# Half steps: a third bank for the first product, packed accumulators, output products three tiles late

## The chip, the cores and the metric

The program runs on one core of a Trainium2 chip. The metric is the device time of one execution in microseconds. The engines are PE (TensorE, matmuls), ACT (ScalarE), DVE (VectorE), POOL (GpSimd) and SP, which here only issues DMAs. Each engine works through its own instruction list in order and waits on semaphores that the others raise.

## The reference, cut to what matters

```
state = 0
for t in range(768):                      # per batch (4) and head (8), head_dim 48
    state = alpha[t][:, None] * state + outer(k[t], v[t])
    y[t] = q[t] @ state
x = y as (3072 tokens, 384)
h = x @ w_in                              # 384 -> 2048
x = (h * cos(h)) @ w_out                  # 2048 -> 384
h = max(x @ w1, x @ w2, x @ w3)           # 384 -> 768
out = h @ w_out2                          # 768 -> 384
```

Everything is float32. Products that need the accuracy are made of three: each operand is split into a high and a low part, and high times high, low times high and high times low are added in PSUM.

## The kernel before

**Tiling.** The sequence is cut into 6 chunks of 128 positions; with 4 batches a chunk has 512 tokens. The attention works in 16 units (4 pairs of heads, 4 batches) for each chunk. The first block of products (h, cos, times `w_out`) goes over 16 tiles of 128 hidden columns for each chunk, and its weights stay in SBUF. The second block follows after the last chunk.

**Half steps.** The attention of chunk c+1 runs beside the products of chunk c. Chunk 0 is special: its products are made in two half steps of 256 tokens each. The first half step (tiles t = 0 to 15) takes the first 256 tokens while the attention units 8 to 15 of chunk 0 and the loading and splitting of the weights still go on; the second (t = 16 to 31) takes the other 256 tokens beside the attention of chunk 1 (`step(0, 0, True, True, True)`). All later steps have 512 tokens for each tile (t = 32 on).

**One tile in a half step.** PE makes `hidden1(t)`: nine matmuls of 256 columns into the bank `h_ps[t % 2]`. ACT then makes `turns` (L558, `turn`), two roundings (L566 and L569, `rounded`), and, after POOL's `frac` (L423), the cosine (L577). DVE multiplies cosine and h into `gated` (L927, `gate`), ACT rounds that to `g_hi` (L584), POOL takes the rest as `g_lo` (L431), and PE makes `accumulate1(t)`: nine matmuls that add to the three output rows `acc[0]`, `acc[1]` (both in `acc_pair`) and `acc[2]` (`acc_last`). `hidden1(t)` waits for `g_done` t-1, that is until gate t-2 has read the bank. PE's list has `accumulate1` two tiles late: hidden(t), accumulate(t-2), then the attention's matmuls of this tile. ACT's list has turn(t), rounded(t), `g_high(t-1)`, cosines(t), and in the first half step a piece of weights (L509) and a copy of states (L517).

**The border between the half steps.** The last accumulates of the first half step (t = 14 and 15) and `stage1(1, 0)` (attention scores of chunk 1) come before hidden(16). Hidden(16) also needs all of x's low part: `x_high0(3)` on ACT (one piece of 96 rows, L529, and three of 32 rows, L537, "quads", two of which ACT makes only after the roundings of tile 15) and `x_low0(3)` on DVE (L860, L874). At the start of the first half step `x_high0(1)` and `x_low0(1)` play the same part, and PE waits for the last of them before hidden(0).

**After the half steps.** ACT copies the three accumulators to `x2` (L721), SP stores it (`spill_x2`). New states of the attention (L839 on DVE) gate the next `stage1` on PE (L1187). SP's list of loads for a chunk a is: queries/keys/decays of pairs 0, 1, 2 (`load_qka`, L270) with the values (`load_v`, L274) between, then the store of x2, then pair 3 and its values.

Of the kernel before, what the change touches and what calls it, by code (L numbers as in the profile page):

```python
# [62 lines left out]
def build(nc, qka, val, wa, wb, spill, out):  # L63
# [8 lines left out]
    with ctx:  # L72
# [47 lines left out]
        with ExitStack() as early:  # L120
# [34 lines left out]
            "mid_state", "y_done", "inc_done", "state_done", "xhi_done", "xlo_done",  # L155
# [24 lines left out]

        def slot(t, half):

            if half:
                tmp, at = t % 2 * HTOK, t // 2 % 2 * HTOK
                return h_ps[t % 2][:, 0:HTOK], slice(tmp, tmp + HTOK), (t % 2, slice(at, at + HTOK)), 2, 4
            bank = last_h[t % 4] if t >= TILES1 * STEPS else h_ps[t % 2]
            return bank[:], slice(0, TOK), (t % 2, slice(0, TOK)), 1, 2
# [75 lines left out]
        def _(sp):  # L263
# [51 lines left out]
            load_qka(1, 3)  # L315
            load_v(1, 2)
            load_v(1, 3)
# [22 lines left out]
            for a in range(2, STEPS):  # L340
                load_qka(a, 0)
                load_v(a, 0)
                load_qka(a, 1)
                load_qka(a, 2)
                load_v(a, 1)
                spill_x2(a - 2)
                load_qka(a, 3)
                load_v(a, 2)
                load_v(a, 3)
            low_ready(sp, POOL_W - 1)  # L350
# [134 lines left out]
        def _(act):  # L485
# [34 lines left out]
            def x_high0(g):  # L520
# [7 lines left out]
                else:  # L528
                    nc.scalar.activation(x_hi[0:PAIR_E, 0, 2, half], y_ps[0:PAIR_E, 0:HTOK],  # L529
                                         ACT.Copy).then_inc(S["xhi_done"], 1)  # L530
                    x_high0_quads(g, (0,))

            def x_high0_quads(g, quads):

                half = slice(g // 2 * HTOK, (g // 2 + 1) * HTOK)
                for j in quads:
                    nc.scalar.activation(x_hi[PAIR_E:P, 0, j, half], y_ps[QUAD * j:QUAD * (j + 1), HTOK:TOK],  # L537
                                         ACT.Copy).then_inc(S["xhi_done"], 1)
# [65 lines left out]
            x_high0_quads(1, (1, 2))  # L604
# [3 lines left out]
            for i in range(TILES1):  # L608
# [11 lines left out]
                if last:  # L620
                    x_high0_quads(3, (1, 2))
# [60 lines left out]

            def step(c, s, attend, prepare_next, half):
                for i in range(TILES1):
# [34 lines left out]
                wait(act, "spilled", 16 * c)  # L719
                for j in range(KT):  # L720
# [48 lines left out]
        def _(dve):  # L769
# [84 lines left out]
            def x_low0_quads(g, quads):  # L854

                half = slice(g // 2 * HTOK, (g // 2 + 1) * HTOK)
                before = g // 2 * (XHI - 1) + g % 2
                for j in quads:
                    dve.wait_ge(S["xhi_done"], before + 2 + j)
                    nc.vector.tensor_tensor(x_lo[0][PAIR_E:P, j, half], y_ps[QUAD * j:QUAD * (j + 1), HTOK:TOK],  # L860
                                            x_hi[PAIR_E:P, 0, j, half].bitcast(fp32), ALU.subtract)

            def x_low0(g):
# [8 lines left out]
                else:  # L872
                    x_low0_quads(g, (1, 2))
                    last = nc.vector.tensor_tensor(x_lo[0][0:PAIR_E, 2, half], y_ps[0:PAIR_E, 0:HTOK],  # L874
                                                   x_hi[0:PAIR_E, 0, 2, half].bitcast(fp32), ALU.subtract)
                    last.then_inc(S["xlo_done"], 1)
# [40 lines left out]
            x_low0_quads(1, (0,))  # L917
# [37 lines left out]
            for i in range(TILES1):  # L955
# [4 lines left out]
                if i == TILES1 - 1:  # L960
                    x_low0_quads(3, (0,))
                elif i in ahead0:
# [5 lines left out]
                if i == TILES1 - 1:  # L968
                    x_low0(3)
                    scan(*ahead0[i])  # L970
# [203 lines left out]
        def _(pe):  # L1174
# [44 lines left out]
            def split_mm(ps, w_at, x_pair, first, final):  # L1219

                xh, xl = x_pair
                mm(ps, w_hi[:, w_at], xh, start=first, stop=False)  # L1222
# [242 lines left out]
```

## Time and profile before

| what | value |
|---|---|
| median of 3 runs | 876.67 us (874.59 to 877.75) |
| the profiled execution's own time | 877.27 us |
| its span (first to last instruction) | 875.3 us |
| PE busy | 832.8 us (95%) |
| DVE, ACT, POOL busy | 69%, 50%, 27% |
| mean granted TensorE clock | 0.988 |
| first half step, hidden(0) to hidden(16) | 33.45 to 99.88 us |
| second half step, hidden(16) to hidden(32) | 99.88 to 161.06 us |

A row of the timeline gives the start, the duration, the engine, the line, what is written and read, and in brackets how long the engine had been idle before and what ended that. Neighbouring matmuls overlap, so starts tell more than durations. The second view of the profile's page cuts the span into 40 slices; after the eighth slice PE stands at 9 tenths or more in every one.

### The profile page before, as it was taken

How to read it: one execution, taken by the hardware profiler on the slowest of the kernel's cores; microseconds unless marked ns; L12 is line 12 of the kernel's file. 1: busy time of each engine (PE TensorE's matmuls, PEld its weight loads, DVE VectorE, ACT ScalarE, POOL GpSimd, SP SyncE). 2: the span in 40 equal slices, each digit the busy share in tenths (PEclk: the TensorE clock that was granted, in tenths of full speed). 3: DMA queues.
4: the chain of work that ended last, by engine and by line, in shares of the span. 5: the costliest groups of instructions: out<-in, count | busy, mean ns of one | idle time of the engine just before them, and what ended most of it. 6: DMA issues, size and time to landing. Idle time of an engine off the chain costs nothing.

```text
span 875.3 us, 15696 instructions
## 1 busy us (share of the span) xinstructions
PE 832.8 (95%) x5446; PEld 759.8 (87%) x5446; DVE 601.6 (69%) x1254; ACT 435.1 (50%) x944; POOL 235.7 (27%) x274
## 2 busy tenths in 40 slices
PE   4687799999999999999999999999999999999998
PEld 4677798888888888888888888889999999999998
DVE  8578588777777777777677457757756566556454
ACT  3686576644454445444544446646343434434333
POOL 6575455333324332333233213310000000000000
PEclk9699899999999999999999999999999999999999
DMA  9632132312321131223123001130101000100001
GB/s 254 178 100 75 35 94 72 113 32 55 82 77 42 55 82 64 55 55 82 64 55 134 3 37 37 40 114 28 38 37 37 37 37 27 31 15 36 1 37 37
DMA packets 13781, 54.36 MB, mean 62 GB/s; under 512 B 1968, under 2 KB 2480, under 8 KB 13712
## 3 DMA queue, kind: packets, MB, share of 16 engines
q1 hardware_dynamic: 12992, 49.55, 19.2%
q0 software_dynamic: 720, 3.93, 1.1%
q8 instruction: 38, 0.62, 0.3%
q14 instruction: 31, 0.25, 0.1%
HBM read 44.04 MB, written 9.44 MB: 61 GB/s over the span
## 4 chain that ended last, share of the span: by engine, by line
PE 48%; DVE 1%; ACT 1%; issue 0%; POOL 0%; DVEq 0%; ACTq 0%
PE h_ps L1315 4%; PE score L1315 4%; PE h_ps L1317 4%; PE h_ps L1316 4%; PE score L1317 4%; PE score L1316 4%; PE h_ps L1222 2%; PE h_ps L1224 2%; PE h_ps L1223 2%; PE acc_pair L1222 2%; PE acc_pair L1223 2%; PE acc_pair L1224 2%; PE acc_pair L1296 1%; PE acc_pair L1295 1%; PE acc_pair L1297 1%; PE acc_last L1224 1%
## 5 line engine op out<-in xcount | busy, mean ns | idle before, releaser
L423 POOL TENSOR_TENSOR work<-work 128x512 f32<-128x512 f32 (+1 forms) x107 | 119.9, 1121 | 307.0 <-DVE work L941 259.3
L577 ACT ACTIVATE work<-work 128x512 f32<-128x512 f32 (+1 forms) x112 | 63.6, 568 | 138.1 <-POOL work L423 131.6
L1222 PE MATMUL h_ps<-x_hi,w_hi 128*128 128x512 f32 (+1 forms) x312 | 121.0, 388 | 5.1 <-DVE work L927 2.7
L927 DVE TENSOR_TENSOR work<-work,h_ps 128x512 f32<-128x512 f32 (+1 forms) x104 | 62.8, 604 | 85.2 <-ACT work L577 84.6
L1224 PE MATMUL h_ps<-x_lo,w_hi 128*128 128x512 f32 (+1 forms) x312 | 113.5, 364 | 0.0
L1223 PE MATMUL h_ps<-x_hi,w_lo 128*128 128x512 f32 (+1 forms) x312 | 113.0, 362 | 0.0
L1222 PE MATMUL acc_pair<-g_hi,w_hi 128*128 128x512 f32 (+1 forms) x224 | 84.2, 376 | 14.6 <-POOL g_lo L431 14.3
L808 DVE RECIPROCAL inv_decay<-decay 112x128 f32<-112x128 f32 x96 | 90.2, 943 | 0.5
L584 ACT ACTIVATE g_hi<-work 128x512 fp32r<-128x512 f32 (+1 forms) x112 | 63.5, 567 | 47.9 <-DVE work L927 42.8
L1224 PE MATMUL acc_pair<-g_lo,w_hi 128*128 128x512 f32 (+1 forms) x224 | 81.7, 365 | 0.0
L1223 PE MATMUL acc_pair<-g_hi,w_lo 128*128 128x512 f32 (+1 forms) x224 | 81.7, 365 | 0.0
L558 ACT ACTIVATE work<-h_ps 128x512 f32<-128x512 f32 (+1 forms) x104 | 54.7, 526 | 48.5 <-PE h_ps L1224 47.6
L480 POOL DMA_DIRECT2D out<-raw x5 | 2.9, 575 | 256.8 <-DVE raw L1117 256.8
L933 DVE TENSOR_TENSOR g_lo<-work,g_hi 128x512 fp32r<-128x512 f32 x80 | 61.9, 774 | 13.9 <-ACT g_hi L584 12.4
L1222 PEld LDWEIGHTS h_ps<-x_hi,w_hi 128*128 128x128 f32 x312 | 60.3, 193 | 12.6 <-DVE work L927 3.1
L1224 PEld LDWEIGHTS h_ps<-x_lo,w_hi 128*128 128x128 f32 x312 | 59.9, 192 | 9.7
L1223 PEld LDWEIGHTS h_ps<-x_hi,w_lo 128*128 128x128 f32 x312 | 60.3, 193 | 7.1
L1222 PEld LDWEIGHTS acc_pair<-g_hi,w_hi 128*128 128x128 f32 x224 | 42.6, 190 | 24.9 <-POOL g_lo L431 15.4
L1315 PE MATMUL h_ps<-x_hi,w_hi 128*128 128x256 f32 x216 | 61.5, 285 | 0.0
L1315 PE MATMUL score<-x_hi,w_hi 128*128 128x256 f32 x216 | 61.4, 284 | 0.0
L1317 PE MATMUL score<-x_lo,w_hi 128*128 128x256 f32 x216 | 60.4, 280 | 0.0
L1317 PE MATMUL h_ps<-x_lo,w_hi 128*128 128x256 f32 x216 | 60.4, 280 | 0.0
(205 smaller groups left out, 2409.5 us busy)
## 6 DMA issues: line engine op xcount, KB each, us to landing
v_all<-val SPq DMA_DIRECT2D x24, 576.0 KB, 3.9
raw<-qka SPq DMA_DIRECT2D x46, 288.0 KB, 5.0
block_out<-x SPq DMA_DIRECT2D x6, 768.0 KB, 3.3
x_in<-block_out SPq DMA_DIRECT2D x6, 768.0 KB, 4.4
raw<-wb SPq DMA_DIRECT2D x12, 384.0 KB, 3.1
out<-raw POOLq DMA_DIRECT2D x5, 768.0 KB, 3.6
stage_own<-wa SPq DMA_DIRECT2D x6, 384.0 KB, 6.8
x<-wa SPq DMA_DIRECT2D x6, 384.0 KB, 5.5
```

Source lines behind the costliest of these rows:

```text
L423: nc.gpsimd.tensor_tensor(frac[:, cols], turns[:, cols], whole[:, cols], ALU.subtract).then_inc(S["frac_done"], 1)
L577: nc.scalar.activation(cosine[:, cols], frac[:, cols], ACT.Sin, scale=TURN).then_inc(S["cos_done"], 1)
L584: nc.scalar.activation(g_hi[:, odd, at], gated[:, cols], ACT.Copy).then_inc(S["ghi_done"], 1)
L808: nc.vector.reciprocal(inv_decay[R, s, b], decay[R, s, b]).then_inc(S["inv_done"], 1)
L927: nc.vector.tensor_tensor(gated[:, cols], cosine[:, cols], h, ALU.mult).then_inc(S["g_done"], 1)
L933: nc.vector.tensor_tensor(g_lo[:, odd, at], gated[:, cols], g_hi[:, odd, at].bitcast(fp32), ALU.subtract).then_inc(S["glo_done"], 1)
L1222: mm(ps, w_hi[:, w_at], xh, start=first, stop=False)
L1223: mm(ps, w_lo[:, w_at], xh, start=False, stop=False)
L1224: return mm(ps, w_hi[:, w_at], xl, start=False, stop=final)
L1315: mm(ps, hi, x_h, start=start, stop=False, skip_group_check=grown)
L1316: mm(ps, lo, x_h, start=False, stop=False, skip_group_check=grown)
L1317: return mm(ps, hi, x_l, start=False, stop=stop, skip_group_check=grown)
```

## The change

1. **Banks.** In a half step hidden(t) no longer alternates between two banks. `half_bank` gives three: `h_ps[0]`, `h_ps[1]` and `acc[2]` in the first half step; `acc[0]`, `h_ps[0]`, `h_ps[1]` from t = 19; t = 16 to 18 alternate between the two `h_ps`. The wait becomes `g_done` t-2 (gate t-3), with t = 17 and 18 as before.
2. **Accumulators.** Half an accumulator is 256 columns, so `half_acc` packs two into a bank: first half step `acc[0]` front and back and `acc[1]` front; second `acc[2]` front and back and `acc[1]` back.
3. **Lateness.** `accumulate1` comes three tiles late, and accumulate(14) and (15) come after hidden(16) and hidden(17).
4. **Copies.** `copy_half(0)` reads the first half step's sums into `x2` on ACT after cosines(18); hidden(19) waits for it (`x2_half`), since it writes `acc[0]`. At the end `copy_half(1)` stands in place of the three copies of 512 columns.
5. **x's parts.** Hidden(0) and hidden(16) wait row by row (`x_row`) for x's low part, no longer for all of it. `x_high0(3)` is made in one go before turn(15), and `x_low0(3)` directly after gate(14).
6. **Loads.** SP's order has pair 3 ahead of the store of x2, and `load_qka(a+1, 0)` ahead of `load_v(a, 3)`, `load_qka(a+1, 1)` ahead of `load_v(a+1, 0)`.

```
+        def half_bank(t):
+            if t < TILES1:
+                return (*h_ps, acc[2])[t % 3]
+            if t < TILES1 + 3:
+                return h_ps[(t + 1) % 2]
+            return (acc[0], *h_ps)[(t - TILES1) % 3]
...
+            def copy_half(part):
+                pair, at = (acc[0], acc[2])[part], slice(part * HTOK, (part + 1) * HTOK)
+                nc.scalar.activation(x2[:, 0:2, at], pair.rearrange("p (j n) -> p j n", j=2), ACT.Copy).then_inc(S["x2_half"], 1)
+                return nc.scalar.activation(x2[:, 2, at], acc[1][:, at], ACT.Copy)
...
+                    if half and i == 2:
+                        act.wait_ge(S["acc_done"], TILES1)
+                        low_ready(act, TILES1 - 1)
+                        copy_half(0).then_inc(S["x2_half"], 1)
...
-                if t < TILES1 * STEPS + 2:
-                    wait(pe, "g_done", t - 1)
+                if t == 2:
+                    pe.wait_ge(S["state_done"], 2 * 6)
+                if t == TILES1 + 3:
+                    pe.wait_ge(S["x2_half"], 2)
+                elif half:
+                    wait(pe, "g_done", {TILES1 + 1: TILES1, TILES1 + 2: TILES1 + 1}.get(t, t - 2))
...
+                    if half and i == 0:
+                        if k < KT - 1:
+                            pe.wait_ge(S["x_row"], (KT - 1) * (t // TILES1) + k + 1)
+                        else:
+                            pe.wait_ge(S["xlo_done"], 2 * (t // TILES1) + 2)
...
-                lag = 2 if attend else 3
+                lag = 3 if half or not attend else 2
...
+                    if half and i < 2:
+                        accumulate1(TILES1 - 2 + i, TILES1 - 2 + i, 0, half)
```

PE's list at the border, before. Rows are in PE's order; `acc_pair<-g_hi` begins an accumulate, `h_ps<-x_hi` a hidden product, `score` is the attention's stage1.

```order
L1187 MATMUL score<-q_dec,k_split 128x128 [waits state_done,mask_done,split_done]
...
L1222 MATMUL acc_pair<-g_hi,w_hi 128x256 [waits glo_done]
...
L1222 MATMUL acc_last<-g_hi,w_hi 128x256
...
L1222 MATMUL h_ps<-x_hi,w_hi 128x256 [waits g_done,xlo_done]
...
L1187 MATMUL score<-q_dec,k_split 128x128 [waits state_done,mask_done]
```

These are stage1(1, 0), accumulate(15) with its third row, hidden(16) and stage1(1, 1). PE's list at the same place now, up to the wait for the copy:

```order
L1234 MATMUL h_ps<-x_hi,w_hi 128x256 [waits xlo_done]
...
L1234 MATMUL acc_pair<-g_hi,w_hi 128x256 [waits glo_done]
...
L1213 MATMUL y_ps<-scores,v_all 96x128 [waits mask_done,xlo_done,v_in0]
...
L1234 MATMUL h_ps<-x_hi,w_hi 128x256 [waits g_done]
...
L1228 MATMUL score<-v_all,scores 112x96 [waits mask_done]
L1234 MATMUL acc_pair<-x_hi,w_hi 128x256 [waits x2_half]
```

Hidden(16), of which the third row's wait is shown, now stands ahead of accumulate(14); hidden(17) follows; and hidden(19), which writes `acc_pair`, has a wait of its own for ACT's copy.

ACT's list around the end of the first half step, before, where x's high parts (`x_hi<-y_ps`) stand against the work of tile 15:

```order
L529 ACTIVATE x_hi<-y_ps 96x256 [waits y_done]
L537 ACTIVATE x_hi<-y_ps 32x256
L558 ACTIVATE work<-h_ps 128x256 [waits cos_done,h_done]
L566 ACTIVATE work<-work 128x256 [waits frac_done,turns_done]
L569 ACTIVATE work<-work 128x256 [waits up_done]
```

and now:

```order
L544 ACTIVATE x_hi<-y_ps 96x256 [waits y_done]
L547 ACTIVATE x_hi<-y_ps 32x256 x3
L568 ACTIVATE work<-h_ps 128x256 [waits cos_done,h_done]
L576 ACTIVATE work<-work 128x256 [waits frac_done,turns_done]
L579 ACTIVATE work<-work 128x256 [waits up_done]
```

All three pieces of 32 rows are now ahead of turn(15).

## Rows read from the trace of the kernel before

**Rows 1.** Waits, whole span, PE: us in total, times, longest.

```profile
PE acc_pair L1222 <- POOL g_lo L431: 14.3, 14, 3.2
```

**Rows 2.** Waits, ACT, both half steps (30 to 160 us).

```profile
ACT work L577 <- POOL work L423: 17.0, 25, 1.6
ACT work L558 <- PE h_ps L1224: 12.8, 11, 4.2
```

**Rows 3.** Timeline, ACT, tile 6: turn and cosine.

```profile
57.17 0.38 ACT L558 ACTIVATE work<-h_ps 128x256 f32<-128x256 f32 x1
...
59.30 0.42 ACT L577 ACTIVATE work<-work 128x256 f32<-128x256 f32 x1 [0.54 <-POOL work L423]
```

**Rows 4.** Timeline, start of the first half step: DVE, PE, POOL, ACT.

```profile
31.68 1.29 DVE L860 TENSOR_TENSOR x_lo<-y_ps,x_hi 32x256 fp32r<-32x256 f32 x3 [1.22 <-ACT x_hi L537]
32.98 0.42 DVE L874 TENSOR_TENSOR x_lo<-y_ps,x_hi 96x256 fp32r<-96x256 f32 x1
...
33.45 0.39 PE L1222 MATMUL h_ps<-x_hi,w_hi 128*128 128x256 f32 x1 [2.40 <-DVE x_lo L874]
...
36.67 0.73 POOL L423 TENSOR_TENSOR work<-work 128x256 f32<-128x256 f32 x1 [1.12 <-ACT work L569]
...
37.43 0.42 ACT L577 ACTIVATE work<-work 128x256 f32<-128x256 f32 x1 [0.84 <-POOL work L423]
```

**Rows 5.** Waits, ACT, 60 to 90 us.

```profile
ACT work L558 <- PE h_ps L1224: 1.3, 2, 0.6
```

**Rows 6.** Timeline, ACT at the border: turn(15), g_high(15), turn(16).

```profile
91.53 0.38 ACT L558 ACTIVATE work<-h_ps 128x256 f32<-128x256 f32 x1
...
96.52 0.42 ACT L584 ACTIVATE g_hi<-work 128x256 fp32r<-128x256 f32 x1 [2.16 <-DVE work L927]
...
102.04 0.38 ACT L558 ACTIVATE work<-h_ps 128x256 f32<-128x256 f32 x1 [4.25 <-PE h_ps L1224]
```

**Rows 7.** Timeline, PE at the border: accumulate(14), hidden(16), hidden(19).

```profile
94.35 0.39 PE L1222 MATMUL acc_pair<-g_hi,w_hi 128*128 128x256 f32 x1 [3.17 <-POOL g_lo L431]
...
99.88 0.41 PE L1222 MATMUL h_ps<-x_hi,w_hi 128*128 128x256 f32 x1
...
109.98 0.36 PE L1222 MATMUL h_ps<-x_hi,w_hi 128*128 128x256 f32 x1
```

**Rows 8.** Busy time by window: PE, PEld, DVE, ACT, POOL, granted clock, DMA.

```profile
95.50:102.30 6.80, 5.64 (x28) 5.38 (x27) 3.48 (x9) 1.47 (x5) 0.72 (x1) 0.50 0.01 4
102.40:109.20 6.80, 6.14 (x57) 5.95 (x56) 5.34 (x14) 5.22 (x16) 5.25 (x8) 1.00 0.00 0
44.30:95.40 51.10, 39.79 (x328) 37.45 (x328) 39.05 (x70) 37.98 (x98) 31.60 (x41) 1.00 0.33 90
```

**Rows 9.** Timeline, ACT: turn(18), cosine(18); and the copies to x2.

```profile
107.46 0.36 ACT L558 ACTIVATE work<-h_ps 128x256 f32<-128x256 f32 x1
...
110.25 0.42 ACT L577 ACTIVATE work<-work 128x256 f32<-128x256 f32 x1
...
161.06 1.09 ACT L721 ACTIVATE x<-acc_pair 128x512 f32<-128x512 f32 x2 [0.99 <-PE acc_last L1224]
```

**Rows 10.** Timeline, PE, second half step: hidden(22), accumulate(20), hidden(23).

```profile
120.48 0.36 PE L1222 MATMUL h_ps<-x_hi,w_hi 128*128 128x256 f32 x1
...
121.63 0.28 PE L1222 MATMUL acc_pair<-g_hi,w_hi 128*128 128x256 f32 x1
...
123.92 0.36 PE L1222 MATMUL h_ps<-x_hi,w_hi 128*128 128x256 f32 x1
```

**Rows 11.** Timeline, stalls of the second half step: PE, DVE, PE; then hidden(32).

```profile
133.78 0.46 PE L1187 MATMUL score<-q_dec,k_split 112*128 112x128 f32 x2 [0.65 <-DVE state L839]
...
134.71 0.77 DVE L792 TENSOR_TENSOR_SCAN decay<-raw,ones 112x63 f32<-112x63 f32 x1 [0.63 <-DMA raw<-qka]
...
158.08 0.39 PE L1222 MATMUL acc_pair<-g_hi,w_hi 128*128 128x256 f32 x1 [1.01 <-POOL g_lo L431]
...
161.06 0.50 PE L1222 MATMUL h_ps<-x_hi,w_hi 128*128 128x512 f32 x1
```

More of the change, by code:

```diff
@@ L179, in banks, with half_acc @@
             return score[n % 2], inc_ps[n % 2], 2, 2
+        def half_bank(t):
[4 more added lines that the diff above has]
+            return (acc[0], *h_ps)[(t - TILES1) % 3]
+        def half_acc(t):
+            front, back = slice(0, HTOK), slice(HTOK, TOK)
+            if t < TILES1:
+                return acc[0][:, front], acc[0][:, back], acc[1][:, front]
+            return acc[2][:, front], acc[2][:, back], acc[1][:, back]
         def slot(t, half):
@@ L338, in load_weights2 @@
                 sp.dma_start(stage2[at], wb[n, at]).then_inc(S[f"stage2_in{at}"], 16)
[L340 to L346, printed above, removed]
+            for a in range(1, STEPS):
                 load_qka(a, 3)
+                if a > 1:
+                    spill_x2(a - 2)
                 load_v(a, 2)
+                if a < STEPS - 1:
+                    load_qka(a + 1, 0)
                 load_v(a, 3)
+                if a < STEPS - 1:
+                    load_qka(a + 1, 1)
+                    load_v(a + 1, 0)
+                    load_qka(a + 1, 2)
+                    load_v(a + 1, 1)
             low_ready(sp, POOL_W - 1)
@@ L530, in x_high0 @@
                                          ACT.Copy).then_inc(S["xhi_done"], 1)
[L531 to L538, printed above, removed]
+                    for j in range(KT):
+                        nc.scalar.activation(x_hi[PAIR_E:P, 0, j, half], y_ps[QUAD * j:QUAD * (j + 1), HTOK:TOK],
+                                             ACT.Copy).then_inc(S["xhi_done"], 1)
             act.wait_ge(S["init_dve"], 1)
@@ L719, in step @@
                 wait(act, "spilled", 16 * c)
+                if half:
+                    copy_half(1).then_inc(S["x2_done"], 1)
+                    return
                 for j in range(KT):
@@ L852, in x_low_quad @@
                     last.then_inc(S["xlo_done"], 1)
[L854 to L861, printed above, removed]
             def x_low0(g):
@@ L871, in x_low0 @@
                                             x_hi[to].bitcast(fp32), ALU.subtract).then_inc(S["xlo_done"], 1)
[L872 to L876, printed above, removed]
+                    return
+                for j in range(KT):
+                    dve.wait_ge(S["xhi_done"], before + 2 + j)
+                    last = nc.vector.tensor_tensor(x_lo[0][PAIR_E:P, j, half], y_ps[QUAD * j:QUAD * (j + 1), HTOK:TOK],
+                                                   x_hi[PAIR_E:P, 0, j, half].bitcast(fp32), ALU.subtract)
+                    if j < KT - 1:
+                        last.then_inc(S["x_row"], 1)
+                nc.vector.tensor_tensor(x_lo[0][0:PAIR_E, 2, half], y_ps[0:PAIR_E, 0:HTOK],
+                                        x_hi[0:PAIR_E, 0, 2, half].bitcast(fp32),
+                                        ALU.subtract).then_inc(S["xlo_done"], 1)
             def low_weights(k):
@@ L1241, in hidden1, with accumulate1 @@
                 last.then_inc(S["h_done"], 1)
-            def accumulate1(t, i, tok, copied, half):
+            def accumulate1(t, i, copied, half):
                 _, _, (odd, at), _, _ = slot(t, half)
@@ L1249, in accumulate1 @@
                     w_at = i * W1COLS + KT * P + j * P
-                    last = split_mm(acc[j][:, tok], slice(w_at, w_at + P), (g_hi[:, odd, at], g_lo[:, odd, at]),
-                                    i == 0, i == TILES1 - 1)
+                    to = half_acc(t)[j] if half else acc[j]
+                    shared = half and j == 1
+                    last = split_mm(to, slice(w_at, w_at + P), (g_hi[:, odd, at], g_lo[:, odd, at]),
+                                    i == 0 and not shared, i == TILES1 - 1, half and j < 2)
                 last.then_inc(S["acc_done"], 1)
@@ L1379, in step @@
                         increment(c + 1, i)
-                if not attend:
+                if lag == 3:
                     accumulate(last - 2)
```

43 lines of the change are left out of this document (17 added, 26 removed).

## The prediction

> **What bounds the kernel now.** I read the engines' busy shares first: PE has 95% of the span, and from the end of the half steps on it is all but continuous. So time can only be won or lost in the first 161 us, and what is won there reaches the end only if the later steps start earlier by it, since they are PE's own work, which the change leaves alone.
>
> In the half steps the waits of PE name POOL's low part in front of an accumulate: 14.3 us in 14 waits [rows 1]. That is what "three tiles late" and "a third bank" aim at. But a wait of PE costs time only where the next thing that PE makes is itself late for somebody. So the second view is ACT's waits: over both half steps ACT waits 17.0 us for POOL's fraction, and 12.8 us for a hidden product [rows 2]. The timeline then shows why these are to be kept apart. In a typical tile of the first half step turn(6) starts at 57.17 and the cosine at 59.30, with 0.54 us of waiting for POOL between [rows 3]: ACT starts a turn, makes two roundings and g_high, waits for the fraction, makes the cosine, then weights and states, and goes straight to the next turn, without any wait for PE. From turn(6) at 57.17 to turn(15) at 91.53 it takes 34.36 us for 9 tiles, 3.8 us each [rows 3, 6]. PE needs for a tile twice nine matmuls, and nine take 1.15 us (121.63 less 120.48), so 2.3 us, and about 0.5 us of attention on average, estimated from the 1.14 that the full attention of a tile takes there (3.44 less 2.3) [rows 10]. So **the first half step is bound by ACT's order with its bubble at POOL**, and the 14.3 us of PE are slack for the most part. The **second half step is bound by PE**: hidden(22) to hidden(23) takes 3.44 us with no idle time [rows 10].
>
> **The change part by part.** Times are those of the profiled execution. I follow hidden(0), turn(15), turn(16), hidden(19) and hidden(32).
>
> *Start.* Before, hidden(0) waits for all of x's low part, until 33.45. The three rows of it are written from 31.68 to 32.97 and the rest by 33.40 [rows 4]. Now two thirds of hidden(0) are made while the last parts are written, and only its last three matmuls follow at 33.45. That brings turn(0) forward by about 1.3 us. POOL had been idle for 1.12 us before its first fraction at 36.67, so it can follow by that much at most, and the cosine at 37.43 moves by 1.05 us or so [rows 4]. Bounds 0 and 1.3, taken **-1.05**.
>
> *First half step.* ACT's order is unchanged up to tile 15, so what goes is its waits for PE: 1.3 us, two of 0.6 [rows 5]; **-1.3**. The rest of PE's 14.3 us brings nothing here. Bounds -0.9 (POOL or DVE is next, see the 0.54) and -2.5 (some of DVE's work, masks above all, moves forward with PE and POOL's fraction comes a little sooner).
>
> *Border.* Turn(15) to turn(16) took 10.51 us (91.53 to 102.04), of which ACT waited 2.16 for gate(15) and 4.25 for hidden(16) [rows 6]. PE had made accumulate(14) at 94.35 after 3.17 us idle, and hidden(16) could only begin at 99.88 [rows 7]. Now hidden(16) stands ahead and is through by about 94. The price: two more quads ahead of turn(15), 0.8 us; but they stood in the place of the wait for the fraction before, so I charge 0.5. Then cosine(15), gate(15) (no longer behind x's low part, a scan and an inverse), g_high(15), states and mid_state follow one another, and turn(16) can start at 96.6 on this scale, 4.65 for that chain after turn(15) plus small gaps. 102.04 - 96.6 = **-5.4**. Bounds -4.25 (only the wait for hidden(16) goes) and -6.4 (both waits go).
>
> *The wait for the copy.* This is the one wait that the change adds. The stretch from turn(16) to turn(18) took 5.42 us, and cosine(18) came 2.79 after turn(18) [rows 6, 9], so cosine(18) comes at 96.6 + 5.65 + 2.8 = 105.05 (with 0.2 for hidden(18), which must await gate(16)). copy_half(0) reads 512 and 256 columns: 512 columns cost 0.55 (1.09 for two [rows 9]), so both some 0.92. Hidden(19) then starts at 105.05 + 0.35 + 0.92 = 106.35, and PE has been idle for about 3 us, since its list to there (hidden 17, 18, accumulate 14, 15 and three units) is done by 103.2. Queued behind it on PE are accumulate(16) and the attention of unit 4; ACT waits for hidden(19) a good 1 us at turn(19). Before, hidden(19) began at 109.98 [rows 7], so PE stands 3.63 us better at hidden(19), of which 5.4 are the border's and -1.8 this wait's: **+1.8**.
>
> *The moved accumulate.* PE had made accumulate(16) before hidden(19); now it has not, and the second half step is PE's: **+1.05** (nine matmuls, 1.15 less the first one's fill [rows 10]).
>
> *The rest of the second half step.* From 109.98 to 161.06 PE was stalled 0.65, 0.54 and 0.67 for new states and 1.01 for the low part of tile 30 (the first and the last are in [rows 11], the other two are like the first). The first and the third stand behind DVE's order (x's low part, then a scan and small operations) and stay. The second came after DVE had waited 0.63 us for a load of keys that SP had queued behind `load_v(1, 3)`; the new order of loads sends it some 5 us earlier, so it goes. The last goes, and about 0.25 comes back, since accumulate(31) still needs its chain from hidden(31). Sum -0.54 - 1.01 + 0.25 = **-1.3**. The last copies to x2 are shorter, 0.92 for 1.65; PE doesn't wait for them: 0. The loads of later chunks pass each other while their own conditions are met tiles earlier: 0.
>
> *The clock.* Right after the longest idle time of PE, the 3.17 us up to 94.35, the granted clock was at half from 95.5 to 102.3; in the 51 us before, with most of PE's other, shorter waits in them, it stayed at 1.00 [rows 1, 7, 8]. The new gap of 3 us ahead of hidden(19) is of that size, and behind it PE is the bound, so every matmul at 1.2 GHz in place of 2.4 counts. A fall of 6.8 us costs half of it, 3.4, none costs 0. The old gap was followed by further waits, the new one by steady work, so I take the middle, a fall half as long: **+1.7**.
>
> Sum: -1.05 - 1.3 - 5.4 + 1.8 + 1.05 - 1.3 + 1.7 = **-4.5**. I round the profiled 877.27 to 872.8; against the median of 876.67 that is **872.2** (the profiled one is 0.6 above the median, well inside the spread of the three). The bounds of the terms together reach from about -9 to +0.
>
> **Rivals.**
>
> (a) *No fall of the clock after the copy's gap*, because three matmul groups of the border stand close together before it. Then the +1.7 goes: 870.5. For it: the gaps from 44.3 to 95.4 cost no clock [rows 8]. Against: the gap of 3.17 did.
>
> (b) *The gain is eaten.* The clock stays at half for 6.8 us as before (+1.7 more) or PE's stalls on new states grow, as the accumulates no longer give DVE time: four sites in the second half step (units 1, 5, 9, 13) of 0.65 where there are three; and the start gives nothing. -4.5 + 1.7 + 1.0 = -1.8: 874.9, no change that can be told (0.3%, 2.6 us, is about what a measurement of this kernel can tell from none).
>
> (c) *DVE becomes the bound of the second half step.* Its order for a unit (new state, gate, scan, inverse, mask) has 5.34 busy of 6.80 in the window after the border [rows 8], 2.7 for 3.44, and PE's stall at 133.78 shows it late once [rows 11]. With PE 4 to 5 us further on and without slack, each DVE delay by POOL's traffic would fall on a stage1. It decides once DVE needs more than 3.44 us for a tile on the mean; at 3.9 the 13 tiles from hidden(19) on give 13 x 0.46 = 6.0 more, and -4.5 + 6.0 = +1.5; with a clock that falls in the gaps (1.7 more): +3.2, 879.9. This is the slower end. Against it: the mean of the trace is 2.7.
>
> (d) *The clock oscillates in the first half step.* With three banks PE runs ahead, then stops at each tile for gate t-3. Its idle time there is the same in sum (11.3 of 51.1 us, [rows 8]). A fall of 6.8 us takes 3.4 x 0.78 (the busy share of that window) = 2.65 us of PE's work, of which PE's slack of 1.0 a tile (3.8 less 2.8) covers 1.8: 0.85 for each. Four falls give +3.4: 875.6. The Trainium skill names this (TensorE: Matmul & The Clock Gate, "A second HAM failure mode: psum-queue depth-cycling"): cycling through PSUM banks lets PE idle briefly so often that the clock goes up and down. By that rule this case would come about; the trace of before, with two banks in turn and a dozen gaps, shows a full clock for 51 us and speaks against it.
>
> (e) *It does more*: masks and gates come earlier and shorten POOL's and ACT's bubbles in the first half step, and there is no fall: -8, 868.7.
>
> **Chances.** The forecast 0.38; (a) 0.22; (b) 0.16; (c) 0.06; (d) 0.06; (e) 0.12. Faster by over 0.3%: the forecast, (a) and (e), and about nothing of the others: 0.72. Within 0.3%: (b) and most of (d): 0.21. Slower: (c) and 0.01 for what I don't see: 0.07. The range runs from 867.5, just beyond (e), to 876.5, which holds (b) and (d), and leaves (c) out.
>
> **What would show each step.** Start: the first hidden product in three pieces, cosine(0) near 36.4. First half step: ACT with no wait for a hidden product, PE's waits moved from the low part to `gated`, turn(15) some 2.3 us earlier less 0.8 for the quads. Border: turn(16) about 5 us after turn(15). Copy: PE idle for about 3 us before a hidden product that writes `acc_pair`, started by ACT's copy; hidden(19) at about 104; a half clock behind it. Second half step: 3.44 us a tile, two stalls on new states, none by a load. Hidden(32) near 156.5. The prediction is wrong if the first half step gets shorter by more than 3 us (then ACT's order was not its bound), if turn(16) comes later than 6.5 us after turn(15), or if the gap before hidden(19) is under 1 or over 5 us.

## The result

The changed kernel takes 870.96 us (median of 20 runs, 870.14 to 877.07), the kernel before 876.12 in the same runs. The ratio is 0.9943, 95% interval 0.9928 to 0.9959: about 5 us faster. The profiled execution has a span of 870.7 us against 875.3.

Five moments of the two traces show where. Times are the starts of the instructions named.

| moment | before | after | the stretch up to it: before, after |
|---|---|---|---|
| cosine(0) | 37.43 | 36.02 | |
| turn(15) | 91.53 | 89.75 | 54.10, 53.73 |
| turn(16) | 102.04 | 93.94 | 10.51, 4.19 |
| hidden(19) | 109.98 | 105.26 | 7.94, 11.32 |
| hidden(32) | 161.06 | 156.15 | 51.08, 50.89 |
| end of the span | 875.3 | 870.7 | 714.2, 714.5 |

The waits of PE over the whole span, after (us in total, times, longest), answer to [rows 1]:

```profile
PE score L1199 <- ACT k_split L559: 18.7, 4, 13.0
PE acc_pair L1234 <- POOL g_lo L446: 2.9, 2, 1.7
PE acc_pair L1234 <- ACT x L694: 2.7, 1, 2.7
...
PE score L1199 <- DVE state L859: 1.9, 5, 0.6
PE h_ps L1234 <- DVE work L942: 1.8, 1, 1.8
```

The kernel before has one wait of the first kind, at the start of the kernel:

```profile
PE score L1187 <- ACT k_split L549: 13.0, 1, 13.0
```

The wait for the low part has shrunk from 14.3 us in 14 waits to 2.9 in 2. Those 11.4 us are not the gain. Half of them came back under another name: PE now runs ahead and stands 5.7 us, in three waits, before attention scores, until ACT has split the keys. The waits of ACT in both half steps answer to [rows 2]:

```profile
ACT work L587 <- POOL work L438: 17.8, 26, 2.0
ACT work L568 <- PE h_ps L1236: 7.2, 9, 1.3
ACT work L568 <- PE acc_pair L1236: 2.5, 3, 1.2
...
ACT work L568 <- PE acc_last L1236: 0.6, 1, 0.6
```

A hidden product now lies in one of three tiles, so its wait has three rows: 10.3 us together for 12.8. The longest was 4.2 and is now 1.3: that is the border. The wait for POOL's fraction is about as large as before, 17.8 for 17.0.

The border, ACT, after (answers to [rows 6]): the quads, turn(15), cosine(15), g_high(15), mid_state, turn(16).

```profile
88.56 1.17 ACT L547 ACTIVATE x_hi<-y_ps 32x256 fp32r<-32x256 f32 x3
89.75 0.38 ACT L568 ACTIVATE work<-h_ps 128x256 f32<-128x256 f32 x1
...
91.87 0.42 ACT L587 ACTIVATE work<-work 128x256 f32<-128x256 f32 x1 [0.53 <-POOL work L438]
92.77 0.42 ACT L594 ACTIVATE g_hi<-work 128x256 fp32r<-128x256 f32 x1 [0.49 <-DVE work L942]
...
93.94 0.38 ACT L568 ACTIVATE work<-h_ps 128x256 f32<-128x256 f32 x1
```

Turn(16) follows without any wait. PE at the same place and at the copy (answers to [rows 7]): first row of hidden(16), accumulate(14), and hidden(19), which now goes into `acc_pair`.

```profile
89.53 0.36 PE L1234 MATMUL h_ps<-x_hi,w_hi 128*128 128x256 f32 x1 [0.22 <-DVE x_lo L886]
```

```profile
92.58 0.39 PE L1234 MATMUL acc_pair<-g_hi,w_hi 128*128 128x256 f32 x1 [1.17 <-POOL g_lo L446]
```

```profile
105.26 0.39 PE L1234 MATMUL acc_pair<-x_hi,w_hi 128*128 128x256 f32 x1 [2.75 <-ACT x L694]
```

And busy time and clock around that (columns as in [rows 8]):

```profile
99.90:106.70 6.80, 4.05 (x37) 3.89 (x36) 5.24 (x13) 4.86 (x13) 3.58 (x6) 1.00 0.40 87
106.80:110.20 3.40, 3.40 (x20) 3.40 (x19) 0.47 (x1) 1.77 (x5) 1.41 (x2) 0.50 0.00 0
110.30:117.10 6.80, 6.80 (x65) 6.80 (x64) 5.91 (x18) 4.60 (x12) 3.54 (x6) 1.00 0.26 89
```

PE stands idle for 2.75 us, and a half clock of 3.4 us follows: 20 matmuls in 3.4 us, where the next window of twice that length has 65.

### The profile page after: what moved, and what is told of

The parts are those of the page before. It is cut to its first block, busy times and chain, and to the rows that moved or that the text cites. A ratio compares the mean times of both kernels' runs of the same rounds, so it can differ in the third digit from the quotient of the medians.

```text
span 870.7 us, 15698 instructions
## 1 busy us (share of the span) xinstructions
PE 832.6 (96%) x5446; PEld 760.9 (87%) x5446; DVE 601.1 (69%) x1254; ACT 435.1 (50%) x945; POOL 236.3 (27%) x274
## 4 chain that ended last, share of the span: by engine, by line
PE 48%; DVE 1%; ACT 1%; issue 0%; POOL 0%; DVEq 0%; ACTq 0%
PE h_ps L1338 4%; PE score L1338 4%; PE h_ps L1340 4%; PE h_ps L1339 4%; PE score L1340 4%; PE score L1339 4%; PE h_ps L1234 2%; PE h_ps L1236 2%; PE h_ps L1235 2%; PE acc_pair L1234 2%; PE acc_pair L1235 2%; PE acc_pair L1236 2%; PE acc_pair L1320 1%; PE acc_pair L1319 1%; PE acc_pair L1318 1%; PE acc_last L1235 1%
## 5 line engine op out<-in xcount | busy, mean ns | idle before, releaser
L1234 PE MATMUL h_ps<-x_hi,w_hi 128*128 128x512 f32 (+1 forms) x282 | 111.9, 397 | 3.8 <-DVE work L942 1.8
L942 DVE TENSOR_TENSOR work<-work,h_ps 128x512 f32<-128x512 f32 (+1 forms) x94 | 58.6, 624 | 81.3 <-ACT work L587 80.9
L1236 PE MATMUL h_ps<-x_lo,w_hi 128*128 128x512 f32 (+1 forms) x282 | 104.7, 371 | 0.0
L1235 PE MATMUL h_ps<-x_hi,w_lo 128*128 128x512 f32 (+1 forms) x282 | 104.2, 370 | 0.0
L568 ACT ACTIVATE work<-h_ps 128x512 f32<-128x512 f32 (+1 forms) x94 | 50.9, 541 | 42.3 <-PE h_ps L1236 41.5
L1234 PEld LDWEIGHTS h_ps<-x_hi,w_hi 128*128 128x128 f32 x282 | 54.2, 192 | 11.6 <-DVE work L942 2.0
L1236 PEld LDWEIGHTS h_ps<-x_lo,w_hi 128*128 128x128 f32 x282 | 53.8, 191 | 9.7
L1339 PE MATMUL h_ps<-x_hi,w_lo 128*128 128x256 f32 x216 | 60.4, 280 | 0.0
L1339 PE MATMUL score<-x_hi,w_lo 128*128 128x256 f32 x216 | 60.4, 280 | 0.0
```

Source lines behind the costliest of these rows:

```text
L942: nc.vector.tensor_tensor(gated[:, cols], cosine[:, cols], h, ALU.mult).then_inc(S["g_done"], 1)
L1234: mm(ps, w_hi[:, w_at], xh, start=first, stop=False, skip_group_check=shared)
L1235: mm(ps, w_lo[:, w_at], xh, start=False, stop=False, skip_group_check=shared)
L1236: return mm(ps, w_hi[:, w_at], xl, start=False, stop=final, skip_group_check=shared)
L1339: mm(ps, lo, x_h, start=False, stop=False, skip_group_check=grown)
```

## The experiments

Theory A is the one of the prediction: the first half step is bound by ACT's order, with its bubble at POOL's fraction; the gain is made at the border; the copy's wait and the half clock behind it give part of it back. Rival B: PE's waits for the low part were the loss, and the third bank and the lateness in the first half step are the gain. Rival C: the second half step is held by DVE's and ACT's chains. Rival D: ACT is only just the bound, POOL or DVE is next.

The table has, for each, the time, the ratio to the kernel before (interval in brackets), and moments of the profiled execution. The first four ran on one chip, the next four on another, the last three on a third.

| kernel | median us | ratio | turn(15) | turn(16) | hidden(19) | hidden(32) | span |
|---|---|---|---|---|---|---|---|
| the change again | 871.56 | 0.9930 [0.9904, 0.9956] | 89.80 | 93.99 | 105.29 | 155.24 | 869.8 |
| two banks in the first half step | 872.45 | 0.9952 [0.9931, 0.9974] | 91.47 | 95.66 | 106.92 | 157.70 | 872.3 |
| old border | 874.39 | 0.9964 [0.9940, 0.9988] | 90.34 | 98.67 | 108.08 | 157.70 | 872.2 |
| early copy | 869.08 | 0.9926 [0.9899, 0.9952] | 90.28 | 94.48 | 101.44 | 151.90 | 866.5 |
| old loads | 873.12 | 0.9962 [0.9947, 0.9977] | 90.75 | 94.94 | 104.73 | 156.95 | 871.4 |
| filled bubble | 867.21 | 0.9900 [0.9872, 0.9929] | 87.04 | 91.24 | 101.03 | 151.86 | 866.1 |
| both | 865.93 | 0.9885 [0.9863, 0.9907] | 87.03 | 91.22 | 98.17 | 149.33 | 863.8 |
| all rows waited for | 872.42 | 0.9950 [0.9936, 0.9964] | 90.47 | 94.67 | 106.00 | 156.08 | 870.6 |
| busy gap | 877.42 | 1.0016 [1.0007, 1.0025] | 88.62 | 92.81 | 104.12 | 153.53 | 875.4 |
| both, again | 867.32 | 0.9889 [0.9872, 0.9907] | 85.82 | 90.01 | 96.95 | 148.11 | 862.4 |
| more filled | 866.75 | 0.9887 [0.9873, 0.9902] | 87.06 | 91.25 | 99.41 | 150.91 | 865.5 |

The moments of one kernel differ from run to run by a us or so, since the clock falls at different moments in the attention ahead of the first half step. Differences between moments of one run are steadier: from hidden(32) to the end all kernels but "busy gap" take 714.2 to 714.6 us. What a kernel wins up to hidden(32) thus reaches the end.

**The change again.**

> The changed kernel once more, as the partner of the others on the same chip. Both theories: 0.9943 of the kernel before, some 5 us faster, with PE idle for 2.5 to 3 us before hidden(19).

It repeats to 0.1 us up to hidden(19), 2.75 us of waiting there included.

**Two banks and two tiles in the first half step, the border as changed.**

```
             if t < TILES1:
-                return (*h_ps, acc[2])[t % 3]
+                return h_ps[t % 2]
...
-                if i >= 3:
-                    accumulate1(i - 3, i - 3, 0, True)
+                if i >= 2:
+                    accumulate1(i - 2, i - 2, 0, True)
```

> The changed kernel with two banks and accumulates two tiles late in the first half step, and the rest of the change kept (hidden(16) and (17) ahead of accumulate(14) and (15), packed accumulators, three banks and three tiles from hidden(19) on). Theory A (the first half step is bound by ACT's order, the gain is made at the border): 0 to 1.3 us slower than the changed kernel, about 871.5. Rival B (the third bank and the later accumulates of the first half step bring the gain, as PE's 14.3 us of waits suggest): 3 us slower or more, 874 and up. Either way PE's waits for the low part in front of an accumulate come back.

Turn(15) comes 1.7 us later than in the run of the changed kernel beside it, although cosine(0) came 0.9 earlier (35.21 for 36.08): the stretch between them takes 56.3 us for 53.7, so it is 2.5 longer. The spans are 2.5 apart and the means of the runs 2.1 (873.1, 871.1), but the medians only 0.9, as the twelve runs spread from 870.7 to 877.4. PE, 30 to 90 us:

```profile
PE acc_pair L1234 <- POOL g_lo L446: 6.8, 10, 1.4
```

The waits for the low part are back (6.8 us in 10; the changed kernel has 1.7 there in 1), and the kernel is some 1 to 2.5 us slower. That lies between theory A's 0 to 1.3 and rival B's 3, and this run alone does not decide between them. ACT has the cost in these rows (same stretch):

```profile
ACT work L587 <- POOL work L438: 11.5, 15, 1.6
ACT state L532 <- PE score L1228: 1.8, 1, 1.8
ACT work L568 <- PE h_ps L1236: 1.7, 3, 0.7
```

3.5 us of waiting for PE, where the changed kernel has 1.2 (below): these 2.3 us make up nearly all of the 2.5. Of PE's waits only the part counts that reaches ACT; that is theory A's kind of term, but larger than its 1.3. It is not what the banks brought over the kernel before, which took 54.1 us for the stretch, or 54.9 with the two quads that the change puts into it. Why two banks are slower here than they were there stays open.

**The old border alone.**

```
+            accumulate1(TILES1 - 2, TILES1 - 2, 0, True)
             stage1(1, 0)
+            accumulate1(TILES1 - 1, TILES1 - 1, 0, True)
...
-                    if half and i < 2:
-                        accumulate1(TILES1 - 2 + i, TILES1 - 2 + i, 0, half)
```

> The changed kernel with the old border alone: accumulate(14), stage1(1, 0) and accumulate(15) again ahead of hidden(16); three banks, row-wise waits, loads and copies as changed. Theory A: the border's 5.4 us come back, less the 1.8 of the copy's wait (the first sums are then ready early and the copy is not late) and the moved accumulate (1.05), so 3 to 5 us slower than the changed kernel, 874 to 876. Rival B: under 1 us slower, 871 to 872.

2.8 us slower than the changed kernel on the same chip, and none of its 12 runs (873.35 to 875.87) reaches the slowest of the other's 7 (871.79). ACT's wait at turn(16) is back at once:

```profile
98.67 0.38 ACT L568 ACTIVATE work<-h_ps 128x256 f32<-128x256 f32 x1 [4.18 <-PE h_ps L1236]
```

Turn(15) to turn(16) takes 8.33 us for 4.19. From turn(16) to turn(18) it takes 5.41 for 7.30, since the half clock at the border now falls into ACT's wait, so 2.25 of the 4.14 us are left at hidden(19). (The 1.05 us of the expectation are not undone by this edit: accumulate(16) still comes after hidden(19).) The loss of 2.8 is a little under the 3 to 5 expected, but more than half of the 5 us gained, and rival B, with under 1, falls.

**The copy ahead of turn(18).**

```
+                    if half and i == 2:
+                        act.wait_ge(S["acc_done"], TILES1)
+                        low_ready(act, TILES1 - 1)
+                        copy_half(0).then_inc(S["x2_half"], 1)
                     turn(t, half)
...
                     cosines(t, half)
-                    if half and i == 2:
-                        ...
```

> The changed kernel with ACT's copy of the first sums moved from behind cosine(18) to ahead of turn(18). Theory A's price for the copy's wait is 1.8 us for the idle time of PE before hidden(19) and 1.7 us for the half clock behind it. If it holds, PE no longer stands still there, the clock stays at full and the kernel gets 3 to 4.5 us faster, 866.5 to 868. Rival C (the second half step is held by DVE's and ACT's chains, not by PE, so that PE's gap is slack): no more than 1 us faster, 870 to 871.

2.5 us faster than the changed kernel by the medians, 3.3 by the spans; three of its ten runs lie at 872.7 to 874.9, so the times alone don't settle it, and the trace has to. The copy is made while ACT would have waited for hidden(18), and hidden(19) starts without a wait:

```profile
99.89 0.57 ACT L693 ACTIVATE x<-acc_pair 128x512 f32<-128x512 f32 x1
100.37 0.37 ACT L694 ACTIVATE x<-acc_pair 128x256 f32<-128x256 f32 x1
100.64 0.38 ACT L568 ACTIVATE work<-h_ps 128x256 f32<-128x256 f32 x1
```

```profile
101.44 0.36 PE L1234 MATMUL acc_pair<-x_hi,w_hi 128*128 128x256 f32 x1
```

Hidden(19) is 3.85 us earlier than in the run beside it, and the half clock behind it is gone. From turn(16) to hidden(19) it takes 6.96 us for 11.30. Not all of that is the copy's: this run has no half clock at the border either, and without it the changed order takes 9.79 ("old loads", "filled bubble"). So the copy's place is worth 2.8 us there. But from there to hidden(32) it takes 50.46 us, no less than the 49.95 of the run beside it, though that had a half clock in it. PE's waits of this kernel, 94 to 155 us:

```profile
PE score L1199 <- DVE state L859: 1.5, 2, 1.1
```

1.5 us of waits for DVE's states came back, 1.1 and 0.4 at 108 and 112 us. So the second half step is PE's, as theory A has it, but with so little to spare on DVE that what the missing half clock gives PE is lost there; there is something in rival C.

**The old order of loads.**

```
-            for a in range(1, STEPS):
-                load_qka(a, 3)
-                if a > 1:
-                    spill_x2(a - 2)
...
+            for a in range(2, STEPS):
+                load_qka(a, 0)
+                load_v(a, 0)
```

> The changed kernel with the old order of loads on SP. Theory: the load of keys for chunk 2 is again queued behind a load of values, DVE waits about 0.6 us for it at the scan in tile 25 and 0.2 in tile 29, and one of PE's stalls on a new state of about 0.5 us comes back: 0.5 us slower than the changed kernel, not to be told by the time (871 to 872), but to be seen in the trace. Rival: the old order is harmless because the loads are early enough when the second half step starts sooner: no such wait.

DVE's waits for the keys are back, and larger:

```profile
130.21 0.78 DVE L812 TENSOR_TENSOR_SCAN decay<-raw,ones 112x63 f32<-112x63 f32 x1 [0.88 <-DMA raw<-qka]
```

```profile
145.72 0.29 DVE L812 TENSOR_TENSOR_SCAN decay<-raw,ones 112x63 f32<-112x63 f32 x1 [1.37 <-DMA raw<-qka]
```

2.2 us for 0.9 in the kernel before. A likely reason, which no run parts from others, is that the queue's condition (increments of later units) stayed where it was while the rest moved forward. PE's waits on new states there are 1.7 us in 2, for 0.6 in 1. Its median is 0.7 us above that of the kernel with all rows waited for on the same chip, which is inside the noise, and 1.6 and 2.2 above the changed kernel's two medians on other chips. The order of loads was worth about 1 us of PE's waits in the trace; hidden(19) to hidden(32) takes 52.2 us, for 50.1 and 50.8 in the two other kernels of this chip that copy late.

**All of x's low part waited for.**

```
                     if half and i == 0:
+                        if k == 0:
+                            pe.wait_ge(S["xlo_done"], 2 * (t // TILES1) + 2)
```

> The changed kernel with hidden(0) and hidden(16) waiting for all of x's low part again, not row by row. Theory from the changed kernel's trace: POOL had no idle time ahead of its first fraction, so hidden(0) up to 1 us later costs nothing or little at the start, and hidden(16) is done some 2.7 us before turn(16) wants it: under 0.5 us slower, 871 to 871.5. Rival (the 1.05 us of the prediction): 1 us slower, 872.

Cosine(0) comes at 36.79 for 36.02 and turn(15) 0.7 us later than in the changed kernel; hidden(32) and the span are the same (156.08 and 870.6 against 156.15 and 870.7). The median is 1 us above the changed kernel's, on another chip. So the row-wise wait brings 0.8 us at its place, and whether any of it reaches the end stays open. Here hidden(0) followed 2.58 us of idle time, and its matmuls start 0.21 us apart at half clock, for 0.12 in the changed kernel.

**The bubble filled.**

```
                 if i:
                     g_high(i - 1, True)
+                if 7 + i < TILES1:
+                    high_weights(7 + i)
                 cosines(i, True)
...
-                if 7 + i < TILES1:
-                    high_weights(7 + i)
```

> The changed kernel with ACT's piece of weights in the first half step moved from behind the cosine to ahead of it, where ACT waits 0.54 us for POOL's fraction. Nothing is added or left out. Theory A (the first half step is bound by ACT's order with this bubble): the bubble goes in nine tiles, so turn(15) comes 3 to 5 us earlier and the kernel gets 3 to 5 us faster, 866 to 868. Rival D (POOL or DVE is next, their decay products, low parts and scans set the pace once ACT is faster): under 1.5 us. Rival B (PE's banks are the bound): no change.

From turn(0) to turn(15) it takes 52.82 us (34.22 to 87.04) against 56.64 (33.11 to 89.75) in the changed kernel: 3.8 less, with the same instructions on every engine. Tile 8 in this kernel:

```profile
57.73 0.40 ACT L594 ACTIVATE g_hi<-work 128x256 fp32r<-128x256 f32 x1
58.04 0.83 ACT L524 ACTIVATE w_hi<-x 128x768 fp32r<-128x768 f32 x1
58.96 0.42 ACT L587 ACTIVATE work<-work 128x256 f32<-128x256 f32 x1
```

The cosine has no wait any more. ACT's waits from 30 to 90 us, first of this kernel, then of the changed one:

```profile
ACT work L587 <- POOL work L438: 6.1, 9, 1.7
ACT g_hi L594 <- DVE work L942: 2.5, 2, 1.3
...
```

```profile
ACT work L587 <- POOL work L438: 11.3, 14, 2.0
ACT work L568 <- PE acc_last L1236: 0.6, 1, 0.6
ACT work L568 <- PE h_ps L1236: 0.4, 1, 0.4
ACT g_hi L594 <- DVE work L942: 0.3, 1, 0.3
ACT state L532 <- PE score L1228: 0.2, 1, 0.2
```

An edit of ACT's list alone takes 5.2 us off its waits for POOL, 2.2 come back as waits for DVE's gates, and turn(15) comes 3.8 earlier. The two profiles of both edits have 52.8 and 53.6 us for the stretch; the seven profiles with three banks and ACT's old order in the first half step have 55.8 to 57.3. That shows ACT's order with its bubble as the bound of the first half step. At the end the kernel is 3.8 us faster than the changed one by the medians and 4.6 by the spans; 1.5 us of the latter come from this profile's full clock at the border.

**Both edits.**

> The changed kernel with both edits, the copy ahead of turn(18) and the weights ahead of the cosine. They act on different stretches, so by theory A the gains add: 6 to 8 us faster than the changed kernel, 863 to 865. Rival D: only the copy's gain, about 868.5.

0.9885 and, on another chip, 0.9889 of the kernel before: 4 to 5 us faster than the changed kernel, where 6 to 8 were expected. The gains of turn(15) (3.8) and of hidden(19) (6.95 us after turn(16), for 9.79 with the bubble alone filled) stand next to each other up to hidden(19); then hidden(19) to hidden(32) takes 51.16 us, with 2.2 us of waits on states. They add less than in full, as with the early copy alone. No kernel here has a lower ratio beyond the noise; it is the version to take.

> The kernel with both edits once more, as the partner of the next one on the same chip: 0.9885 of the kernel before.

**More filled.**

```
                 if i:
                     g_high(i - 1, True)
+                if i - 1 in OUTPUT_AT and i >= 9 and not last:
+                    first_state(OUTPUT_AT[i - 1])
+                if i == 14:
+                    split_keys(1, 0)
```

> Both edits, and from tile 9 on, where no weights are left to fill ACT's wait for the fraction, the copy of states and the split of keys of tile 14 are made ahead of the cosine. Theory A: three or four more bubbles of 0.5 us go, 1 to 2 us faster than both edits alone, as long as ACT's order is the bound of those tiles. Rival D: DVE's gates are late there already (ACT waits 3.0 us for them after the first of the two edits), and the gain is under 0.5 us.

0.9887 against 0.9889 beside it: nothing. Turn(0) to turn(15) is 53.9 us, for 53.6 of "both, again". The time is as rival D has it, the waits are not: from 30 to 90 us ACT waits less for POOL's fraction (5.9 us for 6.8) and for DVE's gates (1.4 for 2.9), and more for hidden products (2.8 for 1.5), with a mean granted clock of 0.88 for 0.91. So ACT's order is no longer the only bound there, and what the next one is stays open.

**The gap filled with work.** 18 matmuls whose result nobody reads.

```
                 if t == TILES1 + 3:
+                    for k in range(18):
+                        mm(acc[2][:, 0:HTOK], w_hi[:, 0:P], x_hi[:, s, 0, tok], start=True, stop=True)
                     pe.wait_ge(S["x2_half"], 2)
```

> The changed kernel with 18 extra matmuls of 256 columns, whose result nobody reads, in PE's gap before hidden(19), just ahead of the wait for the copy. At 0.115 us each they take 2.1 us, so the 2.75 us of waiting stay, filled with work. This parts the wait's own price from the clock's. Theory A (the half clock behind the gap costs 1.7 us, as PE is the bound there): no fall of the clock at 107 us, hidden(19) to hidden(32) 1.0 to 1.7 us shorter, the kernel 1 to 1.7 us faster than the changed one. Rival C (the fall is hidden, DVE's order holds the second half step): the fall goes, PE's waits on new states grow by as much, no change.

PE's rows at the gap:

```profile
101.15 2.30 PE L1244 MATMUL acc_last<-x_hi,w_hi 128*128 128x256 f32 x18
104.12 0.38 PE L1234 MATMUL acc_pair<-x_hi,w_hi 128*128 128x256 f32 x1 [0.67 <-ACT x L694]
```

As expected, 0.67 us of idle time in place of 2.75, and no half clock behind it. Hidden(19) to hidden(32) takes 49.41 us with 0.60 us of stall, against 50.89 with 0.56 and 49.95 with none in the two profiles of the changed kernel. Less the stalls that is 48.8 for 50.3 and 50.0. The same sum holds over all profiles: the five without a half clock there (early copy, both, both again and more filled are the others) come to 48.8 to 49.0, the seven with one to 49.6 to 50.6, on the mean 48.9 and 50.1. **The half clock of 3.4 us cost about 1.2 us**, less than the 1.7 of the prediction. Yet the kernel takes 877.42 us, more than the changed one's 870.96 and the 876.37 of the kernel before on its chip; its 12 runs lie between 875.86 and 878.87. The loss is elsewhere, in the second block of products, 600 us later:

```profile
720.30 0.57 PE L1340 MATMUL score<-x_sums,w_hi 128*128 128x256 f32 x1 [3.71 <-issue]
723.57 0.37 PE L1342 MATMUL score<-x_lo,w_hi 128*128 128x256 f32 x1 [1.84 <-issue]
```

PE stood for 5.55 us and waited for nothing that the trace shows as an instruction of another engine. The section on the hardware comes back to it. The ratio of this run says nothing on the gap; the stretch from hidden(19) to hidden(32) does.

## Why the prediction was right

The forecast was 872.2 us, 4.5 less than before; measured were 870.96 and a ratio that makes 5.0. The main parts of the forecast's mechanism, ACT's order as the bound, the border and the copy's wait, are shown by the runs; that the sum came out so close is luck in part. Step by step, in the profiled executions:

- **Start: -1.05 predicted, -1.41 measured at cosine(0).** x's low part itself was begun 1.04 us earlier (30.64 for 31.68), ahead of anything that the step is about: the clock was at half from 24.8 to 28.2, before from 23.8 to 30.6. Three kernels that begin x's low part as late as before (old loads, filled bubble, both: 31.71 to 31.76) have cosine(0) at 36.31 to 36.37, so the step is worth 1.1. Right. POOL was the limit, as said: it had no idle time left ahead of its first fraction.
- **First half step: -1.3 predicted.** From cosine(0) to turn(15) it is 0.37 less, and 1.17 if the 0.8 us for the two quads is set apart. The size fits, the reason only in part. Of the two waits for a hidden product that were to go, the one at turn(14) went and the one at turn(11) stayed (0.63 us); the rest came from waits for POOL, 0.8 us less. And the seven profiles with this code spread from 53.4 to 54.9 us, where the one profile before has 54.9 with the quads: the gain is 0 to 1.5, and -1.17 is one draw. Of the 11.4 us that PE waits less, at most so much mattered.
- **Border: -5.4 predicted, quads included.** The stretch is 6.3 us shorter, and 5.5 with the quads. Right. Gate(15) no longer stands behind other work (0.49 us of wait for it, 2.16 before), and turn(16) has no wait.
- **The copy's wait: +1.8 predicted, +3.4 measured.** This is the step that was mis-sized. The idle time of 2.75 us before hidden(19) is the foreseen 3. What was not foreseen is that turn(17) and turn(18) waited for their hidden products, 1.15 and 0.57 us: the granted clock was 0.51 from 93.2 to 96.6, where the rest of accumulate(14) and the attention ahead of hidden(17) are made. I had given these PE's full speed. From accumulate(14) to hidden(17) it takes 3.98 us, and 2.39 in "old loads", where the clock stayed at full:

```profile
92.58 0.39 PE L1234 MATMUL acc_pair<-g_hi,w_hi 128*128 128x256 f32 x1 [1.17 <-POOL g_lo L446]
...
96.56 0.37 PE L1234 MATMUL h_ps<-x_hi,w_hi 128*128 128x256 f32 x1
```

```profile
93.58 0.38 PE L1234 MATMUL acc_pair<-g_hi,w_hi 128*128 128x256 f32 x1 [1.18 <-POOL g_lo L446]
...
95.97 0.36 PE L1234 MATMUL h_ps<-x_hi,w_hi 128*128 128x256 f32 x1
```

In that kernel and in "filled bubble" turn(16) to hidden(19) takes 9.79 us, for 11.32 here. The prediction's own steps for it (96.6 to 106.35) make 9.75.
- **The moved accumulate, the stalls and the half clock: +1.05 - 1.3 + 1.7 = +1.45 predicted, -0.2 measured.** The stalls fell from 2.87 to 0.56 us, 1 us more than forecast; the half clock came at its place and for the 3.4 us assumed, and cost about 1.2. This sum came out 1.6 us better than forecast and the step before 1.6 worse: that they cancel is luck.
- **After the half steps: nothing predicted, 0.3 us given back.**

Of the signs named, two did not come: ACT still waits for hidden products in the first half step, at turn(0) and turn(11), and PE's waits went to the splits of keys more than to `gated`. Of the rivals, (a) didn't come: the fall of the clock after the copy's gap was there in both profiles of the changed kernel. Its 870.5 lies nearer to the measured 870.96 than the forecast does, but not for its reason. (b) and (c) didn't come either: PE's stalls on new states shrank to 0.56 us. Nor did (e): the clock fell. (d) came in its ups and downs of the clock, but not in its price. The row of 30 to 90 us, before and then after:

```profile
30.00:90.00 60.00, 46.59 (x358) 43.83 (x357) 43.35 (x75) 43.59 (x112) 40.94 (x54) 0.94 0.35 98
```

```profile
30.00:90.00 60.00, 48.58 (x368) 47.19 (x368) 44.38 (x77) 45.43 (x116) 41.58 (x53) 0.86 0.39 106
```

The granted clock of this stretch fell from 0.94 to 0.86, and yet turn(15) came 1.8 us earlier, 1.4 of it from the start. The Trainium skill (TensorE: Matmul & The Clock Gate, "A second HAM failure mode: psum-queue depth-cycling") warns of such ups and downs with banks in rotation, and of lost throughput. The trace agrees that the clock goes down more, but the kernel with two banks has 0.89 there, so that the third bank is the reason is not shown. The loss of throughput does not show in ACT's pace: of the seven profiles with three banks and ACT's old order, that of the changed kernel had a clock of 0.84 from turn(1) to turn(15) and took 52.7 us, "busy gap" 0.90 and 52.3, "old loads" 0.93 and 53.4. PE runs ahead with three banks and then stands in longer pieces, with a half clock around them:

```profile
66.61 0.79 PE L1199 MATMUL score<-q_dec,k_split 112*128 112x128 f32 x2 [3.10 <-ACT k_split L559]
```

## What to carry to other kernels

A large sum of waits in front of an engine is no loss if the engine behind it never waits for what it makes; look for the engine that has only one wait left in its loop, here ACT with 0.54 us for each tile, and put work into that wait: moving two lines there was worth 3.8 us, beside the 5 of the whole change. At a border between two stages, order the list of the bound engine by who is waited for next, and place a copy that frees a bank where its engine would have waited anyway. A gap at the bound engine costs more than its length if a half clock follows it, here about 1.2 us on top of 2.75. And what one engine wins is kept only as far as the next one has time to spare: with the early copy, waits for DVE's states took back what the full clock gave.

## What the runs showed of the hardware

**Extra instructions can cost time far away.** The kernel with 18 more matmuls lost 5.55 us of PE "issue" at 716 to 724 us, in the second block, whose main part is a loop. The queues that carry instructions tell more. From 700 to 800 us the changed kernel has, in the view of the DMA queues (packets, MB, share):

```profile
q8 instruction: 1, 0.02, 0.1%
```

and the one with the extra matmuls:

```profile
q8 instruction: 8, 0.13, 0.6%
```

So with 18 matmuls more, this queue kept moving while the loop ran, and without them it hardly did. Over the whole span it has 47 packets, and 38 in each of the twelve other profiles; from hidden(32) to the end the kernel takes 721.9 us, for their 714.2 to 714.6. These rows speak for a wait for code as the stall, but do not prove it, nor do they tell why code is loaded again there; no run here varied the count. The half clock behind the stall added to it:

```profile
719.00:726.40 7.40, 4.26 (x18) 4.18 (x19) 0.18 (x1) 0.39 (x1) 0.00 (x0) 0.54 0.02 4
```

For experiments it means that a kernel with work added or taken out is to be compared by stretches of its trace, and that its whole time can mislead, here by 7 us.

**Long gaps and the clock.** PE's waits before hidden(19) were 2.75 us in both profiles of the changed kernel, 2.74 with two banks and with all rows waited for, 2.62 with the old loads and with the bubble filled, and 2.25 with the old border. Each of the seven was followed by about 3.4 us of half clock; with 0.67 us of idle time there (busy gap), or none (early copy, both, both again, more filled), it stayed at full. Shorter waits went either way: behind the 1.17 to 1.19 us before accumulate(14) the clock fell in five profiles (changed, changed again, two banks, busy gap, more filled) and stayed at full in four (old loads, filled bubble, both, both again).
